# Attention and two feed-forward layers: tables that place each visit in tiles two and three, half-width attention sums, and x's high halves multiplied first

## The chip, the cores and the metric

The kernel runs on one core of one Trainium2 chip. The metric is the device time of one execution in microseconds (us), lower is better. The time before is 940.05 us, the median of 3 runs (938.64 to 941.47).

## The reference, cut to what matters

```python
q_d, k_d, v_d = means of q, k, v over groups of 4 positions       # 144 positions
out_d = softmax(q_d k_d^T / 8) v_d                                # pooled attention
out_local = softmax(q k^T / 8 where |i - j| < 4) v                # banded attention
x = repeat(out_d, 4) + out_local                                  # (4, 8, 576, 64) -> (2304, 512)
h = x @ w1_in;  x = (h * sigmoid(h)) @ w1_out                     # layer 1, 512 -> 2048 -> 512
h = x @ w2_in;  out = (s * relu(h)**2 + b) @ w2_out               # layer 2
```

Batch 4, 8 heads, 576 positions, head width 64, all in fp32.

## The kernel before, in words

**Split products.** Each large product is made of three fp32r matmuls per tile of 128 rows of weights: high half of the weights by high half of the data, high by low, low by high (`PASSES`, line 93). The low half is a subtraction (`split_lo`, line 320, a helper used on DVE and POOL).

**Tiles.** Layer 1 is cut into eight tiles of 288 tokens (half a batch), numbered 0 to 7 in the code (so "tile two" of the title is t = 1). A tile is a list of 32 blocks, `BLOCKS`: up 0, up 1, up 2, down 0, up 3, down 1, ..., up 15, down 13, down 14, down 15. An up block is 12 matmuls of 288 columns into `pH[:, f % 2]` (line 764), a down block 12 matmuls into `pY` (line 769). Four blocks are one **slot**, so that a tile has eight slots of 48 matmuls, and a place in a slot is told by the number `k` of the matmul behind which the small work comes. Layer 2 (line 823 up, line 838 down) has four and a half tiles of 512 tokens, without attention.

**What goes with an up block.** PE finishes up f; ACT takes its tanh (`tanh1`, L909); DVE multiplies (`gate1`, L1195; it signals `g_ready`, for which up f + 2 waits, since it reads pH); ACT rounds the high half (`g_high`, L862); POOL subtracts the low half (`g_low`, L320; it signals `g_split`, for which down f waits).

**Attention beside it.** While tile t is multiplied, the input of tile t + 1 is made. In the start and tile 0, a head has transposes of its probabilities (L621, L625), scores (L599, L602) and sums (`attend`, L645 and L649) on PE; in `small` tile 0 puts the transposes behind matmul 9 of a slot, the scores of the next head behind 15 and the sums behind 38. `attend` multiplies with the pair's two heads at once, so the stationary side has 128 columns, of which 64 are this head's. From tile 1 on only the pooled attention uses PE so. The banded part is done by rows: the scores of a head go to DRAM as bands (`store_band`, `read_band`), and when 8 heads' bands are back, one softmax serves all (`row_shift`, `row_exps`, `row_normalise`); POOL multiplies nine rows of probabilities with v (`weigh`, L1530), DVE sums each (`sum_row`, L1301), PE turns the sums in three groups of three (`turn`, L694), ACT puts a group into x (`place`), DVE adds the pooled part (`x_add`, L1311), ACT rounds the high half (`x_round`) and POOL makes the low half (`x_low`, signals `x1_ready`).

**A visit** is what PE does for one head from tile 1 on (`small_rows`): transposes of the head before, scores of this one, and at each odd head the sums of an earlier pair (`attend_pair`, L663). DVE then takes the maximum (`maxima`), ACT the exponentials and a copy of the scores into the one staging buffer `s_sb` (`exps`), DVE normalises. Tile 1 has 12 visits, tile 2 has 10, tiles 3 to 5 have 8.

**What sets the order.** Every engine runs its own list in order, written out by hand: `UNITS_IN` says which heads a slot of tiles 1 and 2 visits (two per slot in tile 1's first four slots), `TWO_UNITS` at which places (7 and 31), `SOFTMAX_IN` the slot of the row softmax (4 in tile 1), `WEIGH_IN` and `SUM_IN` the slots of the rows, `TURNS_IN` slot and place of the three turns (in tile 1 behind matmuls 36 of slot 6, 2 and 47 of slot 7). In tile 1's last slot (`late`) the steps place, x_add, x_round and x_low stand behind everything else of the tile. Up 0 of a tile waits for `x1_ready` before each chunk of x. The SP queue issues the loads and stores in an order of its own.

## Time and profile before

| what | us |
|---|---|
| median of 3 runs | 940.05 (938.64 to 941.47) |
| the profiled execution's own time | 939.28 |
| its span, first to last instruction | 937.5 |
| its mean granted TensorE clock | 0.998 |
| PE busy | 923.5 (99%) |
| POOL, DVE, ACT busy | 460.6 (49%), 439.5 (47%), 372.8 (40%) |

A busy share counts from an instruction's start to its end; the ends of matmuls are modelled, and consecutive ones overlap. So PE's 99% does not say that PE never waited, and the length of a stage is taken below from starts to starts.

### The profile page before, as it was taken

What the parts mean: (1) busy time and instruction counts of PE and PEld (TensorE: products, weight loads), DVE (VectorE), ACT (ScalarE), POOL (GpSimd) and SP (SyncE); (2) the same over time, 40 slices, a digit from 0 to 9 for tenths busy, and PEclk for the clock granted to TensorE, in tenths of its full rate; (3) what the DMA queues carried; (4) which work ended last, traced back from release to release, by engine and by line L of the source; (5) the groups of instructions that cost most, each with busy time, mean ns of one, the idle gap of its engine ahead of it and who ended that gap; (6) DMA issues with size and microseconds to landing.
All of it is one profiled execution on the core that took longest, in us unless ns stands there. A gap on an engine that the chain in (4) does not pass through costs nothing.

```text
span 937.5 us, 15634 instructions
## 1 busy us (share of the span) xinstructions
PE 923.5 (99%) x5969; PEld 852.0 (91%) x5969; DVE 439.5 (47%) x909; ACT 372.8 (40%) x999; POOL 460.6 (49%) x444
## 2 busy tenths in 40 slices
PE   8999999799999999999999999999999999999998
PEld 8999999799999999999999988888888888888897
DVE  5577436657556566564655642233224222322232
ACT  5666343344534545445345632232224223322332
POOL 7778457859777687685662222213222222222222
PEclk9999999999999999999999999999999999999999
DMA  6756353343442532523006520010002000100000
GB/s 167 196 156 183 76 145 88 84 123 75 96 105 66 136 72 53 143 62 64 22 25 220 162 95 1 1 58 33 0 1 89 0 0 0 67 0 0 35 11 23
DMA packets 87170, 68.75 MB, mean 73 GB/s; under 512 B 38720, under 2 KB 73024, under 8 KB 87104
## 3 DMA queue, kind: packets, MB, share of 16 engines
q1 hardware_dynamic: 86944, 67.71, 27.2%
q8 instruction: 42, 0.69, 0.3%
q14 instruction: 24, 0.20, 0.1%
q10 hardware_dynamic: 160, 0.15, 0.1%
...
## 4 chain that ended last, share of the span: by engine, by line
PE 87%; DVE 5%; ACT 3%; POOL 3%; issue 1%; DMA 1%; ACTq 0%; POOLq 0%; DVEq 0%
PE pH L823 21%; PE pY L838 21%; PE pH L764 17%; PE pY L769 16%; PE pS L599 3%; PE pS L602 2%; PE pO L663 1%; DVE w_in_hl L320 1%; POOL weighted L1530 1%; DMA stage_in<-w_in 1%; PE pO L625 1%; PE pO L649 1%; DVE w_out_hl L320 1%; PE pY L782 1%; POOL g_hl L320 1%
## 5 line engine op out<-in xcount | busy, mean ns | idle before, releaser
L320 POOL TENSOR_TENSOR g_hl<-act,g_hl 128x288 fp32r<-128x288 f32 (+2 forms) x208 | 200.0, 962 | 440.8 <-ACT g_hl L862 440.2
L769 PE MATMUL pY<-g_hl,w_out_hl 128*128 128x288 f32 x1536 | 236.7, 298 | 2.6 <-POOL g_hl L320 2.6
L764 PE MATMUL pH<-x_hl,w_in_hl 128*128 128x288 f32 x1518 | 228.6, 297 | 3.8 <-POOL x_hl L320 3.2
L769 PEld LDWEIGHTS pY<-g_hl,w_out_hl 128*128 128x128 f32 x1536 | 212.0, 188 | 3.5 <-POOL g_hl L320 3.3
L764 PEld LDWEIGHTS pH<-x_hl,w_in_hl 128*128 128x128 f32 x1518 | 209.1, 188 | 4.8 <-issue 3.1
L823 PE MATMUL pH<-x_hl,w_in_hl 128*128 128x512 f32 (+1 forms) x960 | 208.4, 368 | 0.0
L838 PE MATMUL pY<-w_out_hl,g_hl 128*128 128x512 f32 x864 | 207.8, 390 | 0.0
L823 PEld LDWEIGHTS pH<-x_hl,w_in_hl 128*128 128x128 f32 x960 | 169.0, 188 | 31.1
L838 PEld LDWEIGHTS pY<-w_out_hl,g_hl 128*128 128x128 f32 x864 | 161.2, 188 | 33.1 <-POOL g_hl L320 0.3
L1417 DVE TENSOR_TENSOR act<-act 128x512 f32<-128x512 f32 (+1 forms) x80 | 55.5, 694 | 270.6 <-ACT act L1102 270.6
L862 ACT ACTIVATE g_hl<-act 128x288 fp32r<-128x288 f32 (+2 forms) x208 | 104.0, 500 | 191.2 <-DVE act L1419 103.7
L1102 ACT ACTIVATE act<-pH 128x512 f32<-128x512 f32 (+1 forms) x80 | 44.3, 554 | 166.0 <-PE pH L823 165.5
L1530 POOL TENSOR_TENSOR weighted<-p_rows,v_loc 128x896 f32<-128x896 f32 x54 | 91.2, 1692 | 3.2 <-issue 2.1
L909 ACT ACTIVATE act<-pH 128x288 f32<-128x288 f32 x128 | 52.8, 412 | 99.7 <-PE pH L764 99.5
L1195 DVE SCALAR_TENSOR_TENSOR act<-act,pH 128x288 f32<-128x288 f32 x128 | 57.5, 449 | 60.7 <-ACT act L909 59.1
L1301 DVE TENSOR_REDUCE g_gap<-weighted 128x128 f32<-128x896 f32 x36 | 64.3, 1790 | 10.8 <-POOL weighted L1530 10.7
L1484 POOL TENSOR_TENSOR vd_f<-vd_f 72x512 f32<-72x512 f32 x32 | 41.6, 1300 | 6.8 <-DMA vd_f<-vp 6.8
L599 PE MATMUL pS<-qk_f 128*96 128x102 f32 x360 | 43.8, 258 | 0.0
L1419 DVE TENSOR_SCALAR act<-act,sb_col 128x512 f32<-128x512 f32 (+1 forms) x80 | 41.6, 520 | 2.9
L1469 POOL TENSOR_TENSOR pair<-qk_f 128x580 f32<-128x580 f32 x31 | 36.2, 1167 | 5.5 <-DMA qk_f<-qk 3.0
L599 PEld LDWEIGHTS pS<-qk_f 128*96 128x96 f32 x360 | 37.7, 167 | 0.0
L1127 DVE TENSOR_REDUCE pS<-pS 72x1 f32<-72x144 f32 x48 | 14.9, 310 | 44.7 <-PE pS L602 44.7
(141 smaller groups left out, 763.0 us busy)
## 6 DMA issues: line engine op xcount, KB each, us to landing
...
```

What stands on the lines that cost most here:

```text
L320: eng.tensor_tensor(lo, full, hi.bitcast(F32), ALU.subtract).then_inc(signal, 1)
L599: pe.matmul(work(n).s_loc[:, j, :], qk_f[:, buf, q0:q0 + TQ], qk_f[:, buf, c:c + KW], start=not masked_by_pe(n) and j == 0, stop=True, ski ...
L764: last = pe.matmul(pH[:, f % 2, 0:T1], w_in[:, wp, c, f * P:(f + 1) * P], x1[:, par, mp, c, :], start=c + n == 0, stop=c == C - 1 and n == 2)
L769: last = pe.matmul(pY[:, c, 0:T1], w_out[:, wp, f, c * P:(c + 1) * P], g_hl[:, f % RING, mp, 0:T1], start=f + n == 0, stop=f == NF - 1 and ...
L823: last = pe.matmul(pH[:, f % 2, 0:T], w_in[:, wp, c, f * P:(f + 1) * P], x2_hl[:, xp, c, 0:T], start=c + n == 0, stop=c == C - 1 and n == 2)
L838: last = pe.matmul(pY[:, j, :], g_hl[:, f % RING, gp, j * P:(j + 1) * P], w_out[:, wp, f, :], start=f + n == 0, stop=f == NF - 1 and n == 2)
L862: return sc.activation(dst, src, ACT.Copy)
L909: sc.activation(act1[:, f % RING, :], pH[:, f % 2, 0:T1], ACT.Tanh, scale=0.5).then_inc(L[0].t_ready, 1)
L1195: ve.scalar_tensor_tensor(act1[:, f % RING, :], act1[:, f % RING, :], 1.0, pH[:, f % 2, 0:T1], ALU.add, ALU.mult).then_inc(L[0].g_ready, 1)
L1301: ve.tensor_reduce(o_row[i].rearrange("p (h d) -> p h d", h=2), weighted[:, i % 2].rearrange("p (h r d) -> p h d r", h=2, r=NR), AX.X, ALU ...
L1417: ve.tensor_tensor(g, g, g, ALU.mult).then_inc(squared, 1)
L1530: gp.tensor_tensor(weighted[:, i % 2].rearrange("p (h r d) -> p h r d", h=2, r=NR), p_rows[:, i, :].rearrange("p (h r) -> p h r", r=NR).un ...
```

## The change

It does the following; all on the same engines and with the same amount of mathematics.

- Tables (`PLACES_IN`, `QK_PAIRS_IN`, `V_PAIRS_IN`, `SOFTMAX_IN`, `WEIGH_IN`, `SUM_IN`, `TURNS_IN`) give each visit, pair sum, weighed row and turn of tiles 1 and 2 a place. Tile 1's slot 0 visits three heads (behind matmuls 2, 20 and 38), its slot 3 one; the row softmax of tile 1 is at the end of slot 3; turns are groups of 3, 4 and 2 rows in all tiles. One v pair sum passes from tile 1 to tile 2.
- ACT takes the exponentials of a visit before it evacuates a pair.
- `first_up`: up 0 of tiles 1 to 7 multiplies all four high chunks of x with the high weights, then with the low weights, and then the low chunks; `early_ups_end` does the same for the last chunk of tile 0's first two ups, and head 8's sums come right behind it.
- In tile 0 transposes and scores stand together behind matmul 11; `attend` of heads 8 to 15 has only this head's 64 columns on the stationary side and writes partitions 0 to 63. Tanh and gate of ups 0 and 1 are taken together.
- In tile 7, layer 2's up 0 (`up2(0, 0)`) stands ahead of the last down block. ACT waits for `g_split` of all of layer 1 before layer 2's first relu.
- SP issues the v loads behind the band's store instead of ahead of the band's read, and does not ask twice for the same pair.

```diff
-UNITS_IN = {1: [(1, 2), (3, 4), (5, 6), (7, 8), (9,), (10,), (11,), (12,)],
+UNITS_IN = {1: [(1, 2, 3), (4, 5), (6, 7), (8,), (9,), (10,), (11,), (12,)],
...
-SOFTMAX, SOFTMAX_IN = 1, {1: 4, 2: 2}
+SOFTMAX, SOFTMAX_IN = (1, 1), {1: (3, 2), 2: (2, 0)}
...
-GROUP = 3
+GROUPS = ((0, 1, 2), (3, 4, 5, 6), (7, 8))
...
-TURNS_IN = {1: {(6, 36): 0, (7, 2): 1, (7, 47): 2}, 2: {(5, 36): 0, (6, 36): 1, (7, 12): 2}}
+TURNS_IN = {1: {(5, 40): 0, (7, 4): 1, (7, 32): 2}, 2: {(5, 36): 0, (6, 36): 1, (7, 17): 2}}
...
+PLACES_IN = {(1, 0): (2, 20, 38), (1, 1): (9, 34), (1, 2): (8, 31), (1, 3): (17,), (1, 4): (21,),
...
-TRANS_AT, SCORES_AT, ATTEND_AT, LAST_ATTEND_AT, FIRST_ATTEND_AT = 9, 15, 38, 34, 23
+TURN_AT, ATTEND_AT, LAST_ATTEND_AT = 11, 38, 34
...
+HIGH_FIRST = [(0, 0), (1, 0), (0, 1)]
...
+                            if w := unit(h, k + (QK_AHEAD if alone else QK_AHEAD + 1)):
+                                load_qk(w)
                             if w := unit(h, k - 1):
                                 read_band(w)
                             if w := unit(h, k):
                                 store_band(w)
...
+                            if u < H - 1 and (w := unit(h, k + V_AHEAD.get(t, 1))):
+                                load_v(w)
+                        if not alone and len(units(t, u + 1)) == 1:
+                            load_v(unit(h, now[-1] + 1))
...
-                        last = pe.matmul(o.outs[:, HALF:HALF + DQ], vd_s[:, buf, k].rearrange("p h d -> p (h d)"),
-                                         o.pdT[:, k, :], start=k == 0, stop=k == 1, skip_group_check=True)
+                        last = pe.matmul(o.outs[0:D, HALF:HALF + DQ], vd_s[:, buf, k, u % 2], o.pdT[:, k, :],
+                                         start=k == 0, stop=k == 1, skip_group_check=True)
+                    elif not startup(n):
+                        j = k - 2
+                        last = pe.matmul(o.outs[0:D, j * TQ:(j + 1) * TQ], v_f[:, buf, j, u % 2],
+                                         o.pT[:, j * TQ:(j + 1) * TQ], start=False, stop=True, skip_group_check=True)
...
+                def first_up(t, par, h):
+
+                    pe.wait_ge(L[0].g_ready, t * NF + 1)
+                    for n, (wp, mp) in enumerate(HIGH_FIRST):
+                        for c in range(C):
+                            if n == 0 and t == 1:
+                                pe.wait_ge(x_hi, c + 1)
+                            elif n == 0:
+                                pe.wait_ge(x_high, C * (t - 2) + c + 1)
+                            if mp:
+                                pe.wait_ge(x1_ready, C * t + c + 1)
...
+                        if t == N1 - 1 and b == len(BLOCKS) - 1:
+
+                            pe.wait_ge(l.g_ready, s + 2)
+                            up2(0, 0, True, T2)
...
-                    for f in ups[:1]:
+                    together = len(ups) if u == 0 else 1
+                    for f in ups[:together]:
                         tanh1(t, f)
...
+                    if u and any(softmax_in(t, u - 1)[1:]):
                         row_normalise(t, h)
...
+                    if behind:
+                        row_shift(t, h)
```

The same work in the order of the instructions, at three places. The rows give line, operation, output and inputs.

PE in a slot of tile 0 (`pO<-ident` are transposes, `pS` scores, `pO<-pdT` and `pO<-pT` the head's sums), before:

```order
L764 MATMUL pH<-x_hl,w_in_hl 128x288 x10
L621 MATMUL pO<-ident,prob 102x96 x3
L625 MATMUL pO<-ident,prob_d 72x72 x2
L764 MATMUL pH<-x_hl,w_in_hl 128x288 x2
L769 MATMUL pY<-g_hl,w_out_hl 128x288 x4
L599 MATMUL pS<-qk_f 96x102 x3
L602 MATMUL pS<-d_f 72x144
L769 MATMUL pY<-g_hl,w_out_hl 128x288 x8
L764 MATMUL pH<-x_hl,w_in_hl 128x288 x12
L769 MATMUL pY<-g_hl,w_out_hl 128x288 x3
L645 MATMUL pO<-pdT,vd_sum 128x72 x2
L649 MATMUL pO<-pT,v_f 128x96 x3
```

and with the change:

```order
L828 MATMUL pH<-x_hl,w_in_hl 128x288 x12
L666 MATMUL pO<-ident,prob 102x96 x3
L670 MATMUL pO<-ident,prob_d 72x72 x2
L644 MATMUL pS<-qk_f 96x102 x3
L647 MATMUL pS<-d_f 72x144
L833 MATMUL pY<-g_hl,w_out_hl 128x288 x12
L828 MATMUL pH<-x_hl,w_in_hl 128x288 x12
L833 MATMUL pY<-g_hl,w_out_hl 128x288 x3
L690 MATMUL pO<-pdT,vd_sum 64x72 x2
L694 MATMUL pO<-pT,v_f 64x96 x3
```

The scores have joined the transposes, so the large matmuls are broken off twice in a slot and not three times, and the sums write 64 partitions instead of 128.

PE at the seam of tiles 1 and 2 (`pO<-ident,act` is the last turn), with the semaphores that it waits for, before:

```order
L769 MATMUL pY<-g_hl,w_out_hl 128x288 x11
L694 MATMUL pO<-ident,act 128x128 [waits rows_placed,rows_summed,pT_copied,o_copied]
L694 MATMUL pO<-ident,act 128x128
L694 MATMUL pO<-ident,o_last 128x128
L764 MATMUL pH<-x_hl,w_in_hl 128x288 [waits x1_ready,g_ready1]
L764 MATMUL pH<-x_hl,w_in_hl 128x288 x2
L764 MATMUL pH<-x_hl,w_in_hl 128x288 [waits x1_ready]
L764 MATMUL pH<-x_hl,w_in_hl 128x288 x2
L764 MATMUL pH<-x_hl,w_in_hl 128x288 [waits x1_ready]
L764 MATMUL pH<-x_hl,w_in_hl 128x288
L663 MATMUL pO<-pdT,vd_sum 128x144 [waits vd_summed,o_copied,pT_copied,rows_placed]
```

and with the change:

```order
L833 MATMUL pY<-g_hl,w_out_hl 128x288 x11
L795 MATMUL pH<-x_hl,w_in_hl 128x288 [waits x_high,g_ready1]
L795 MATMUL pH<-x_hl,w_in_hl 128x288 [waits x_high] x3
L795 MATMUL pH<-x_hl,w_in_hl 128x288 x4
L714 MATMUL pO<-pdT,vd_sum 128x144 [waits vd_summed,o_copied,pT_copied,rows_placed]
L714 MATMUL pO<-pdT,vd_sum 128x144
L670 MATMUL pO<-ident,prob_d 72x72 [waits pT_copied,probs_ready]
L670 MATMUL pO<-ident,prob_d 72x72
L644 MATMUL pS<-qk_f 96x102 [waits probs_ready,qkd_summed]
L644 MATMUL pS<-qk_f 96x102 x2
L647 MATMUL pS<-d_f 72x144
L795 MATMUL pH<-x_hl,w_in_hl 128x288 [waits x1_ready] x4
```

The last turn is gone from the seam (it stands 15 matmuls earlier), and eight matmuls and a whole visit now come before the first that waits for a low half.

POOL in tile 1 around the first weighed rows (`vd_f`, `vd_sum` a pair sum of v; `pair`, `d_f` one of q and k; `g_hl` is `g_low`), before:

```order
L1484 TENSOR_TENSOR vd_f<-vd_f 72x4x128
L1488 TENSOR_TENSOR vd_sum<-vd_f 72x2x2x64
L320 TENSOR_TENSOR g_hl<-act,g_hl 128x288
L1469 TENSOR_TENSOR pair<-qk_f 128x580
L1473 TENSOR_TENSOR d_f<-pair 128x290
L1530 TENSOR_TENSOR weighted<-p_rows,v_loc 128x896
L320 TENSOR_TENSOR g_hl<-act,g_hl 128x288
L1530 TENSOR_TENSOR weighted<-p_rows,v_loc 128x896 x2
L320 TENSOR_TENSOR g_hl<-act,g_hl 128x288
L1484 TENSOR_TENSOR vd_f<-vd_f 72x4x128
L1488 TENSOR_TENSOR vd_sum<-vd_f 72x2x2x64
L1530 TENSOR_TENSOR weighted<-p_rows,v_loc 128x896
```

and with the change:

```order
L337 TENSOR_TENSOR g_hl<-act,g_hl 128x288
L1576 TENSOR_TENSOR vd_f<-vd_f 72x4x128
L1580 TENSOR_TENSOR vd_sum<-vd_f 72x2x2x64
L1622 TENSOR_TENSOR weighted<-p_rows,v_loc 128x896
L337 TENSOR_TENSOR g_hl<-act,g_hl 128x288
L1622 TENSOR_TENSOR weighted<-p_rows,v_loc 128x896 x2
L337 TENSOR_TENSOR g_hl<-act,g_hl 128x288
L1622 TENSOR_TENSOR weighted<-p_rows,v_loc 128x896
L337 TENSOR_TENSOR g_hl<-act,g_hl 128x288
L1622 TENSOR_TENSOR weighted<-p_rows,v_loc 128x896 x2
L337 TENSOR_TENSOR g_hl<-act,g_hl 128x288
L1622 TENSOR_TENSOR weighted<-p_rows,v_loc 128x896
```

No pair sum stands between the weighed rows any more, and they begin at the start of slot 4 instead of near its end.

## Rows read from the trace of the kernel before

**Rows 1.** Windows of tiles 0 to 3 and 7: span, length, busy by engine, clock, DMA.

```profile
43.70:110.50 66.80, 66.26 (x538) 65.79 (x538) 47.08 (x141) 38.68 (x126) 48.37 (x45) 1.00 0.50 140
...
110.50:182.70 72.20, 66.74 (x535) 65.12 (x534) 42.32 (x97) 29.70 (x99) 49.31 (x49) 1.00 0.48 112
182.70:250.30 67.60, 66.57 (x514) 65.18 (x515) 39.91 (x85) 30.05 (x96) 51.54 (x52) 0.97 0.36 85
250.30:311.50 61.20, 61.20 (x492) 61.10 (x491) 37.43 (x77) 28.15 (x85) 46.48 (x46) 1.00 0.39 92
...
488.00:540.70 52.70, 51.41 (x387) 50.95 (x386) 29.95 (x49) 31.06 (x70) 13.70 (x17) 1.00 0.58 181
```

**Rows 2.** Timeline of PE in tile 1: starts of blocks in slots 4 to 6.

```profile
145.87 1.75 PE L764 MATMUL pH<-x_hl,w_in_hl 128*128 128x288 f32 x12
...
152.05 1.74 PE L769 MATMUL pY<-g_hl,w_out_hl 128*128 128x288 f32 x12
153.63 1.76 PE L764 MATMUL pH<-x_hl,w_in_hl 128*128 128x288 f32 x12
...
160.91 1.76 PE L764 MATMUL pH<-x_hl,w_in_hl 128*128 128x288 f32 x12
```

**Rows 3.** Timeline of PE: three waits, in brackets idle us and releaser.

```profile
49.54 1.59 PE L764 MATMUL pH<-x_hl,w_in_hl 128*128 128x288 f32 x10 [0.51 <-DVE act L1195]
...
182.72 0.64 PE L764 MATMUL pH<-x_hl,w_in_hl 128*128 128x288 f32 x3 [2.91 <-POOL x_hl L320]
...
538.98 1.20 PE L769 MATMUL pY<-g_hl,w_out_hl 128*128 128x288 f32 x7 [1.02 <-POOL g_hl L320]
```

**Rows 4.** Window behind the seam of tiles 1 and 2: granted clock third from the end.

```profile
186.00:188.00 2.00, 2.00 (x13) 2.00 (x12) 0.19 (x1) 0.00 (x0) 0.86 (x2) 0.50 0.00 0
```

**Rows 5.** Timeline of PE in tile 0: a head's sums, a short run, scores.

```profile
90.88 0.56 PE L645 MATMUL pO<-pdT,vd_sum 72*128 72x72 f32 x4
...
91.92 1.43 PE L769 MATMUL pY<-g_hl,w_out_hl 128*128 128x288 f32 x9
...
94.86 0.51 PE L764 MATMUL pH<-x_hl,w_in_hl 128*128 128x288 f32 x2
95.21 0.69 PE L769 MATMUL pY<-g_hl,w_out_hl 128*128 128x288 f32 x4
95.74 0.69 PE L599 MATMUL pS<-qk_f 128*96 128x102 f32 x6
96.26 0.41 PE L602 MATMUL pS<-d_f 128*72 128x144 f32 x2
```

**Rows 6.** Timelines of ACT and DVE at the seam of tiles 1 and 2.

```profile
179.85 0.85 ACT L862 ACTIVATE x_rows<-pO 128x384 f32<-128x384 f32 x1 [3.62 <-PE pO L694]
181.22 1.18 ACT L862 ACTIVATE x_hl<-x_rows 128x288 fp32r<-128x288 f32 x3 [0.52 <-DVE x_rows L1311]
...
180.73 2.16 DVE L1311 TENSOR_TENSOR x_rows<-x_rows,g_gap 128x288 f32<-128x288 f32 x4 [1.44 <-ACT x_rows L862]
```

**Rows 7.** POOL and DVE by form in tile 1: count, busy us, mean ns.

```profile
L1530 POOL TENSOR_TENSOR weighted<-p_rows,v_loc 128x896 f32<-128x896 f32 x9 | 15.1, 1693 | 1.0 <-DVE p_rows L1294 1.0
L320 POOL TENSOR_TENSOR g_hl<-act,g_hl 128x288 fp32r<-128x288 f32 x16 | 12.8, 803 | 16.7 <-ACT g_hl L862 16.6
...
L1301 DVE TENSOR_REDUCE g_gap<-weighted 128x128 f32<-128x896 f32 x6 | 10.5, 1780 | 2.1 <-POOL weighted L1530 2.0
```

**Rows 8.** Timeline of DVE: the row softmax's subtraction in tiles 1 and 3.

```profile
149.93 2.42 DVE L1282 TENSOR_TENSOR e_rows<-e_rows,act 128x126 f32<-128x126 f32 x1
...
263.95 0.40 DVE L1282 TENSOR_TENSOR e_rows<-e_rows,act 128x126 f32<-128x126 f32 x1
```

**Rows 9.** Transfers that touch score_bands in tile 1's first slots.

```profile
DMA to landing us min/median/max: 2.2/3.0/4.2
```

**Rows 10.** Timelines of ACT and POOL: layer 2's first relu and first low half.

```profile
543.61 0.60 ACT L1102 ACTIVATE act<-pH 128x512 f32<-128x512 f32 x1 [2.33 <-PE pH L823]
...
546.33 1.29 POOL L320 TENSOR_TENSOR g_hl<-act,g_hl 128x512 fp32r<-128x512 f32 x1 [7.41 <-ACT g_hl L862]
```

More of the change, by code:

```diff
@@ L962, in slot @@
                         exps(w)
-                    for f in ups[1:]:
+                    for f in ups[together:]:
                         tanh1(t, f)
@@ L1006, in slot_rows @@
                 def slot_rows(t, h, u):
-                    now = units(t, u)
+                    ahead, before, between, after = visits(t, u)
+                    within, at_end, behind = softmax_in(t, u)
                     here = groups(t, u)
-                    two = len(now) == 2
                     finish = u == H - 1 and not late(t, u)
@@ L1017, in slot_rows @@
                         y_out1(t - 1)
+                    for v in ahead:
+                        visit(h, v)
                     f, more = UPS[u][0], UPS[u][1:]
@@ L1021, in slot_rows @@
                         x_round(t, h, 0)
-                    if two:
-                        pooled(h, now[0])
-                        exps(unit(h, now[0]))
+                    for v in before:
+                        visit(h, v)
                     g_high(L[0], t, f, 2, T1)
-                    if u == softmax_in(t) != SOFTMAX:
+                    if within:
                         row_exps(t, h)
@@ L1327, in slot_rows @@
                         x_add(t, h, 0)
-                    if two:
-                        maxima(unit(h, now[0]))
+                    for v in ahead:
+                        maxima(unit(h, v))
+                        normalise(unit(h, v))
+                    for v in before:
+                        maxima(unit(h, v))
                     gate1(t, UPS[u][0])
-                    if u == softmax != SOFTMAX:
+                    for i in sums[1]:
+                        sum_row(t, i)
+                    if within:
                         row_shift(t, h)
```

247 lines of the change are left out of this document (140 added, 107 removed), and 8 rows, old and new, of tables (QK_PAIRS_IN, V_PAIRS_IN).

## The prediction

> **What bounds the kernel now.** The busy times (table above) come first: PE is at work for 99% of the span, no other engine for half of it, so time is only won where PE's own work shrinks or where PE waits. The windows by tile come next [rows 1]. The reader is to see that tile 3 takes 61.2 us and tile 7 52.7, but tile 1 takes 72.2 and tile 2 takes 67.6. To know what they should take, I price a slot from starts [rows 2]. A down block of 12 large matmuls takes 153.63 - 152.05 = 1.58 to 1.59 us, so a slot of four is 6.36. Slot 4, with a visit and a pair's sums, takes 153.63 - 145.87 = 7.76; slot 5, with a visit alone, takes 7.28. So a visit costs 0.92 and a pair's sums 0.48. Tile 1 has 4 visits and one pair more than tile 3: 61.2 + 3.68 + 0.48 = 65.4, and it takes 72.2, so **6.8 us** are lost. Tile 2 has 2 visits and one pair more, 63.5, and takes 67.6: **4.1 us** lost. Tile 7 has 32 blocks only, 50.9, and takes 52.7: **1.8 us**. Tile 0 has one wait of note, 0.51 us [rows 3].
>
> The waits on PE's timeline say where [rows 3]. The largest is 2.91 us at the seam of tiles 1 and 2, for the low half of x, from POOL. Behind it the granted clock falls: a window of 2 us from 186 on has 0.50, the 1.2 GHz level [rows 4]; PE had stood still for 2.91 us before. Over all of tile 2 the clock is 0.97 [rows 1], so 67.6 x 0.03 = 2.0 us of full speed are lost to it, counted within tile 2's 4.1. The rest of tile 1's loss is many small waits and two of 1 us or so in its last slot, where POOL is late. The last large one is 1.02 us before tile 7's last block, for POOL's low half of g [rows 3]. Such a row understates a wait by some 0.15 us, since the end of the matmul before is modelled late.
>
> **The change part by part.**
>
> *Tile 0.* A head's sums take 91.92 - 90.88 = 1.04 us for ten instructions (each fp32 matmul counts twice), 104 ns each, with 72 or 96 columns streamed and 128 columns of weights [rows 5]. The scores stream more, 102 columns, over 96 columns of weights, and take (96.26 - 95.74) / 6 = 87 ns [rows 5]. So the wide weights set the pace, not the stream. With 64 columns of weights the six of 96 streamed columns should take at most 87 ns, and the four of 72 about 87 x 72 / 102 = 61: 0.77 us, 0.27 saved. Bounds: nothing, if something fixed holds it at 104 ns, and 0.5 us, if half the weights meant half the time. I take 0.27, since the scores' row is nearest. Eight heads, all on PE's path: **2.2 us** (0 to 4).
>
> By the Trainium skill (TensorE: Matmul & The Clock Gate, section LDWEIGHTS), a load's time goes with its columns, at 1.2 per ns: 107 ns for 128 and 53 for 64. The 107 agrees with the 104 here; taken alone, the rule would give 0.5 us a head, 4 us in all, and a sum 1.9 us better than mine. I stay with the row, since it counts the stream too.
>
> Breaking off the large matmuls costs something: two of them take 95.21 - 94.86 = 0.35 us where 0.265 is their share [rows 5], so each return costs 0.085. One return fewer in seven slots: **0.6 us**. The scores move 4 matmuls forward and the transposes 2 back; DVE's copy of the transposed probabilities now comes after up f instead of beside it, but the gate behind it is due two blocks later, so that costs nothing. Tanh and gate of ups 0 and 1 are taken together, ahead of head 9's maxima: the 0.51 us (0.66 real) goes. Late next is up 2, with only head 8's shortened sums as cover for tanh and gate of up 0; I leave 0.25 us there. **0.4 us** net. Tile 0: 3.2 us.
>
> *Tile 1.* Nine rows cost POOL 1.69 us each and DVE 1.78, and a `g_low` 0.8 [rows 7]. Before, they shared slots 4 to 7 with three pair sums of 2 us. Now slots 4 and 5 hold seven rows and no pair sum: POOL has 3 x 1.69 + 2 x 0.8 = 6.7 and 4 x 1.69 + 1.6 = 8.4 us for slots of 7.3 to 8.1, and 6.9 in slot 6; `g_low` is due four blocks (6.4 us) after its up, so the excess is hidden. DVE has three sums, 5.3 us, in each of slots 5 and 6, and beside them at most 2.7 us: tile 3's 37.4 busy us less nine sums, over eight slots [rows 1, 7]. That is 8.0 for slots of 7.6 and 7.8, but the gates are due two blocks (3.2 us) later. What is late next: the q and k sum of head 12, last in slot 6 on POOL, about 0.3 us; and slot 0, where three visits stand 18 matmuls apart, 2.4 + 0.9 = 3.3 us. Each visit must copy its scores into the one staging buffer after the store of the last has landed, median 3.0, up to 4.2 us [rows 9]. I leave 0.6 us there. Some 0.2 more for other small waits: 1.1 us.
>
> *The seam of tiles 1 and 2.* Before, from the last turn ACT's place took 0.85 us from 179.85, then x_add, x_round and x_low held PE to 182.72 [rows 3, 6]. The last turn has moved from behind matmul 47 to behind 32, 15 matmuls or 2.0 us earlier, and places two rows, not three. From the turn, place (an estimate of 0.65 for two rows), x_add (2.16 / 4 = 0.54) and x_round (0.45) [rows 6] with signals bring the first high chunk after 2.1 us: PE comes then. The four high chunks follow each other at 0.5 us, PE needs 0.13 each: about 1.1 us of waiting in small pieces. Then come four matmuls without a wait and a visit with a pair's sums, 1.9 us, under which POOL makes the low halves. I take **1.3 us** for the seam, (0.5 to 3), and no fall of the clock, because no single stop is near 2.9 us; tile 7, with its stop of 1.02, has a clock of 1.00 [rows 1].
>
> *Tile 2.* The visits are spread (7, 31, then 9, 40), and the last turn stands at 17 instead of 12; 0.4 us of small waits stay. So of 6.8 + 4.1 = 10.9 us of loss, 1.1 + 1.3 + 0.4 = 2.8 remain: **8.1 us** saved.
>
> *Tile 7.* Up 0 of layer 2 takes 2.7 us and covers the last `g_low`: **1.1 us**. The last down block now ends later against layer 2's first relu, but the relu still has two up blocks (5.4 us) before down 0 needs it; the chain from relu to the end of `g_low` takes 546.33 + 1.29 - 543.61 = 4.0 us [rows 10]. Covered, with the relu waiting for ACT's four copies of y first.
>
> *Tiles 3 to 6.* `first_up` changes nothing where x is ready. Group two now turns four rows, so place is about 0.3 us longer, hidden by the 15 matmuls (2 us) before the next turn. The v loads stand behind the band's store, some 4 us later in a slot, and are read in the next one. The SP queue's other waits stay. Cost nothing; if these covers failed, a few tenths per tile.
>
> The sum: 3.2 + 8.1 + 1.1 = **12.4 us**. The profiled execution took 939.28 us (span 937.5), so the changed one should take 926.9; the median of the runs shown is 0.8 above it, so 940.05 - 12.4 = **927.7 us**.
>
> **The rivals.**
>
> *POOL blocks the row softmax and the weighed rows slide.* The same subtraction took 0.40 us in tile 3 and 2.42 in tile 1, where POOL ran without a pause [rows 8]. The change puts it at the end of slot 3, where a v pair sum follows `g_low` on POOL. SP also issues the read of band 7 only behind a v load that waits for POOL's pair sum in slot 3. If both add up to 4 us, rows and turns slide by as much and the seam opens again: about 4 us of the 8.1 are lost, **931.7 us**. Against: `g_low`'s slack takes up the first 2 us, which I counted. The Trainium skill (SBUF — State Buffer, Who interferes with whom) says that a DVE instruction with two SBUF inputs and a POOL one that reads SBUF exclude each other for a whole instruction, which is what these rows look like and speaks against placing it there.
>
> *The clock falls at the seam again*, because four short stops act as a long one: 2.0 us stay, **929.7**.
>
> *The narrow weights bring nothing*: a fixed cost per fp32 pass, 2.2 us stay, **929.9**.
>
> *Slower.* The row softmax stands in DVE's list ahead of slot 4's gates. If band 7 lands late, everything on DVE waits, and with it PE's ups, one for one. Expected is landing before slot 4 begins; slack is about 4 us. To end 2.8 us above the time before it would have to cost 15 us, landing 19 us late. That decides it, and with landings of 2.2 to 4.2 us [rows 9] it would need a queue of four or five of them in series on SP. Then **943 us** or more.
>
> **How the numbers follow.** Forecast 0.63, POOL 0.13, clock 0.11, weights 0.07, slower 0.03, and 0.03 for a change whose tables mostly fail, with only tile 0 and tile 7 kept and new waits, near the old time. A measurement can tell 0.3%, 2.8 us, from no change: faster is under 937.2. So faster 0.94, same 0.03, slower 0.03. The range: the best end takes a seam of 0.5 and 1 us more from the weights and small waits, 924.7; the upper one holds POOL's case with 2 us of tile 0 lost too, 933.7.
>
> **What would show it.** Right: tile 0 at 63.6 us with a head's sums near 0.77; tile 1 near 66.5, tile 2 near 65; no wait of PE over 1 us at the seam, clock 1.00 in it; tile 3 still 61.2; no wait before tile 7's last down. Wrong: waits for `prob_d` in slot 0, a subtraction of over 2 us that moves the first weighed row behind 5 us of slot 4, or a seam of over 2 us.

## The result, and the profile after

The changed kernel takes 933.05 us (median of 4 runs, 932.34 to 933.89). The kernel before took 940.76 us in the 4 runs made beside it (938.64 to 941.55). The ratio is 0.9932, with a 95% interval of 0.9917 to 0.9947. So it is faster: the medians differ by 7.7 us, and the interval of the ratio stands for 5.0 to 7.8 us, where 12.4 were forecast. The profiled execution took 932.44 us with a span of 930.6, 6.9 us less than the span of before.

Where did the rest of the 12.4 us go? The starts of PE's first matmul of each tile answer it. Tile 0 counts from its first matmul behind the start-up (43.70 us before, 43.57 after); tile 7 ends where layer 2's first down block starts.

| stretch, us | before | after | difference | forecast |
|---|---|---|---|---|
| tile 0 | 66.81 | 68.09 | +1.28 | -3.2 |
| tiles 1 and 2 | 72.21 + 67.57 | 66.75 + 64.91 | -8.12 | -8.1 |
| tiles 3 to 5 | 61.20, 61.22, 61.22 | 61.86, 61.86, 61.84 | +1.92 | 0 |
| tile 6 | 54.05 | 54.05 | 0 | 0 |
| tile 7 | 60.87 | 59.10 | -1.77 | -1.1 |
| start-up, and layer 2 from its first down block | 432.4 | 432.1 | -0.2 | 0 |

The same windows as in [rows 1], of the changed kernel (columns as there: span, then busy of PE, PEld, DVE, ACT and POOL, clock, DMA share, GB/s):

```profile
43.57:111.66 68.09, 65.73 (x541) 63.03 (x539) 51.75 (x142) 37.57 (x126) 47.93 (x46) 1.00 0.51 143
111.66:178.41 66.75, 66.34 (x536) 65.23 (x534) 39.15 (x96) 30.30 (x98) 46.53 (x46) 1.00 0.41 102
178.41:243.32 64.91, 64.59 (x513) 63.61 (x514) 39.99 (x86) 30.90 (x98) 52.55 (x53) 1.00 0.42 104
243.32:305.18 61.86, 61.45 (x492) 61.11 (x490) 37.73 (x79) 28.66 (x87) 48.71 (x49) 1.00 0.37 91
```

Tile 2's clock is back at 1.00 (0.97 before). DVE is busy 51.75 us in tile 0, 4.7 more than before, with one instruction more: its instructions got longer. The timeline of PE shows the waits that are left (in brackets idle us and releaser):

```profile
68.63 0.43 PE L666 MATMUL pO<-ident,prob 96*102 96x96 f32 x3 [0.93 <-DVE x_f L1263]
87.43 0.43 PE L666 MATMUL pO<-ident,prob 96*102 96x96 f32 x3 [1.42 <-DVE x_f L1263]
178.41 1.94 PE L795 MATMUL pH<-x_hl,w_in_hl 128*128 128x288 f32 x8 [0.20 <-ACT x_hl L938]
303.49 1.85 PE L833 MATMUL pY<-g_hl,w_out_hl 128*128 128x288 f32 x12 [0.41 <-POOL g_hl L337]
```

The 2.91 us at the seam [rows 3] are 0.20 now, and the 1.02 us before tile 7's last block are gone. New are two waits in tile 0 (2.35 us together, about 0.15 more for each in fact, as in the prediction) and one of 0.32 to 0.41 before the last down block of tiles 2 to 5. Follow the 1.42 back: the transposes wait for DVE's `x_f`, and DVE is late from here on:

```profile
75.21 0.45 DVE L1263 TENSOR_TENSOR x_f<-pO,o_down 64x288 f32<-64x288 f32 x1 [0.62 <-ACT o_down L938]
75.70 3.42 DVE L1269 CAST x_hl<-x_f 128x288 fp32r<-128x288 f32 x1
79.15 0.86 DVE L337 TENSOR_TENSOR x_hl<-x_f,x_hl 128x288 fp32r<-128x288 f32 x1
```

The same cast takes 0.31 to 0.73 us at its three other places. POOL's timeline over the same stretch has no pause between its first four instructions, and one of 0.07 us (78.95 to 79.02) ahead of the fifth:

```profile
74.54 1.29 POOL L337 TENSOR_TENSOR w_out_hl<-stage_out,w_out_hl 128x512 fp32r<-128x512 f32 x1
75.79 0.80 POOL L337 TENSOR_TENSOR g_hl<-act,g_hl 128x288 fp32r<-128x288 f32 x1
76.56 1.28 POOL L337 TENSOR_TENSOR w_out_hl<-stage_out,w_out_hl 128x512 fp32r<-128x512 f32 x1
77.80 1.15 POOL L1561 TENSOR_TENSOR pair<-qk_f 128x580 f32<-128x580 f32 x1
79.02 0.67 POOL L1565 TENSOR_TENSOR d_f<-pair 128x290 f32<-128x290 f32 x1
```

The cast ended at 79.12, just behind that pause. Before, POOL had a gap of 0.26 us at 75.3 there and one of 0.62 behind its `g_low`, and the cast took 0.31.

The sums of a head, on PE and on its weight loads (PEld), beside [rows 5]:

```profile
54.68 0.56 PE L833 MATMUL pY<-g_hl,w_out_hl 128*128 128x288 f32 x3
55.16 0.47 PE L690 MATMUL pO<-pdT,vd_sum 72*64 72x72 f32 x4
55.47 0.66 PE L694 MATMUL pO<-pT,v_f 102*64 102x96 f32 x6
56.06 1.46 PE L833 MATMUL pY<-g_hl,w_out_hl 128*128 128x288 f32 x9
```

```profile
55.16 0.32 PEld L690 LDWEIGHTS pO<-pdT,vd_sum 72*64 72x64 f32 x4 [0.17 <-issue]
58.81 0.34 PEld L666 LDWEIGHTS pO<-ident,prob 96*102 96x102 f32 x3
```

From 55.16 to 56.06 the ten instructions take 0.90 us, not 0.77. The three large matmuls ahead take 0.48, not the 0.39 of the kernel before: the first load of 64 columns comes only when its matmul is due, with 0.17 us in which PEld does nothing. The second group of narrow loads, at 55.41, is ahead of its matmul (55.47) again. The load of the 102-column transposes, at 58.81, comes 0.13 us ahead of its matmul at 58.94.

### The profile page after: what moved, and what is told of

It reads as the page before. It is cut to its first block, busy times and chain, and to the rows that moved or that the text cites. A ratio compares the mean times of both kernels' runs of the same rounds, so it can differ in the third digit from the quotient of the medians.

```text
span 930.6 us, 15634 instructions
## 1 busy us (share of the span) xinstructions
PE 920.2 (99%) x5969; PEld 847.5 (91%) x5969; DVE 440.2 (47%) x909; ACT 372.9 (40%) x999; POOL 460.1 (49%) x444
## 4 chain that ended last, share of the span: by engine, by line
PE 85%; POOL 5%; DVE 3%; issue 2%; ACT 2%; DMA 1%; SPq 1%; ACTq 0%; POOLq 0%; DVEq 0%
PE pH L897 21%; PE pY L912 21%; PE pY L833 16%; PE pH L828 16%; PE pS L644 3%; POOL weighted L1622 2%; POOL g_hl L337 1%; PE pS L647 1%; PE pH L795 1%; PE pO L714 1%; POOL vd_f L1576 1%; PE pY L856 1%; PE pO L670 1%; POOL vd_sum L1580 1%; DVE act L1276 0%
## 5 line engine op out<-in xcount | busy, mean ns | idle before, releaser
L828 PE MATMUL pH<-x_hl,w_in_hl 128*128 128x288 f32 x1428 | 212.2, 296 | 0.0
L897 PEld LDWEIGHTS pH<-x_hl,w_in_hl 128*128 128x128 f32 x960 | 169.0, 188 | 30.9
L828 PEld LDWEIGHTS pH<-x_hl,w_in_hl 128*128 128x128 f32 x1428 | 196.1, 188 | 0.2 <-DVE act L1276 0.2
L946 ACT ACTIVATE pS<-pS,stats 72x144 f32<-72x144 f32 x60 | 20.7, 345 | 43.0 <-DVE stats L1211 32.5
```

What stands on the lines that cost most here:

```text
L828: last = pe.matmul(pH[:, f % 2, 0:T1], w_in[:, wp, c, f * P:(f + 1) * P], x1[:, par, mp, c, :], start=c + n == 0, stop=c == C - 1 and n == 2)
L897: last = pe.matmul(pH[:, f % 2, 0:T], w_in[:, wp, c, f * P:(f + 1) * P], x2_hl[:, xp, c, 0:T], start=c + n == 0, stop=c == C - 1 and n == 2)
```

## The experiments

Lengths of tile 0 are counted in this section from the start of up 2, the one mark that is the same in all kernels; by it the kernel before has 64.89 us and the change 66.18. The table has the profiled executions (us); "net" is tile 0 less its listed waits, each counted 0.15 us longer than its row says. For the kernel before, with its one wait of 0.51, the net is 64.23. e7, e8 and e9 also have e3's edit, and e12 is e9 with one more.

| kernel | tile 0 | net | tiles 1 + 2 | tile 3 | tile 7 | time, median |
|---|---|---|---|---|---|---|
| the change | 66.18 | 63.53 | 131.66 | 61.86 | 59.10 | 933.05 |
| e1, groups of 3, 3, 3 | 65.96 | 63.54 | 132.90 | 61.18 | 60.04 | 932.99 |
| e2, wide weights | 64.90 | 64.26 | 132.25 | 61.84 | 60.17 | 932.87, one run |
| e3, ACT casts | 63.48 | 63.48 | 132.39 | 61.86 | 60.06 | 931.68 |
| e4, split | 66.02 | 63.89 | 131.93 | 61.84 | 61.26 | 934.77, one run |
| e5, halves mixed | 65.02 | 63.52 | 136.07 | 61.86 | 61.20 | 937.17, one run |
| e6, mask first | 65.71 | 63.55 | 131.84 | 61.87 | 60.97 | 933.12, one run |
| e7, 72 columns | 61.88 | 61.39 | 131.60 | 61.87 | 59.11 | 929.73, one run |
| e8, cast and groups | 63.49 | 63.49 | 131.77 | 61.22 | 59.10 | 928.39 |
| e9, e8 and 72 columns | 61.90 | 61.39 | 131.67 | 61.18 | 60.80 | 926.00 |
| e10, reduction | 64.99 | 63.51 | 131.70 | 61.85 | 60.03 | 932.30, one run |
| e11, last turn later | 64.93 | 63.53 | 133.46 | 61.86 | 60.22 | 934.07, one run |
| e12, x later | 61.86 | 61.36 | 131.98 | 61.18 | 60.56 | 928.40 |

**e1: groups of three rows again.**

```diff
-GROUPS = ((0, 1, 2), (3, 4, 5, 6), (7, 8))
+GROUPS = ((0, 1, 2), (3, 4, 5), (6, 7, 8))
```

> The changed kernel with turns of 3, 3 and 3 rows again; all else stays. Theory: the group of four rows makes ACT's place 1.18 us long instead of 0.9, so that tanh, g_high and g_low of up 14 start about 0.4 us later, POOL gives the last low half 0.66 us later, and PE waits 0.41 us (0.56 real) before the last down block. Then tiles 3 to 5 (61.86 us each) go back to 61.2, the wait before their last down block is gone, tile 2 gains 0.5 too, the seam of tiles 1 and 2 loses up to 0.3 since the last group has three rows again: 2.2 us less in all, with a ratio to the kernel before near 0.991. Rival, the v loads that stand behind the band's store are the cause: tiles 3 to 5 stay at 61.8 and the time stays within 0.3 us.

Tiles 3 to 5 took 61.18, 61.23 and 61.22: the theory for them holds, and the v loads are cleared. The chain shows in both timelines. The copy of the four rows pushes tanh of up 14 to 296.73, 53.41 us into tile 3, where e1 has it at 52.99, and the last low half ends 0.67 us later in the tile (60.11 us into it, against 59.44). The rows are place and that low half, of the change and then of e1:

```profile
295.78 1.18 ACT L938 ACTIVATE x_rows<-pO 128x512 f32<-128x512 f32 x1 [1.46 <-PE pO L744]
302.43 1.00 POOL L337 TENSOR_TENSOR g_hl<-act,g_hl 128x288 fp32r<-128x288 f32 x1
```

```profile
296.79 0.91 ACT L938 ACTIVATE x_rows<-pO 128x384 f32<-128x384 f32 x1 [1.35 <-PE pO L744]
302.89 1.02 POOL L337 TENSOR_TENSOR g_hl<-act,g_hl 128x288 fp32r<-128x288 f32 x1
```

But the whole kernel gained nothing (932.99): with three rows in the last turn the seam waits 0.23 + 0.57 us, and tile 2's last down block 0.55, so tiles 1 and 2 took 1.2 us more, not 0.2 less as I had summed; tile 7 took 0.9 more, for a reason of its own (below). The two groupings suit different tiles.

**e2: wide weights again.**

```diff
-    o.outs[0:D, j * TQ:(j + 1) * TQ], v_f[:, buf, j, u % 2], ...
+    o.outs[:, j * TQ:(j + 1) * TQ], v_f[:, buf, j].rearrange("p h d -> p (h d)"), ...
```

(the same for `vd_s`, and ACT and DVE read the head's own rows)

> The changed kernel with the sums of heads 8 to 15 over 128 columns of weights again. Theory: the narrow weights bring 0.90 instead of 1.04 us a head, but the first narrow load stands 0.17 us idle behind the 128-column ones and the three matmuls ahead of it take 0.48 instead of 0.39, so 0.06 us a head and 0.4 to 0.5 us in eight heads: tile 0 gets 0.4 to 0.5 us longer (68.5), a slot without waits 8.65 instead of 8.59. Rival, the forecast's own price, whose gain only hides behind late DVE work in tile 0: 0.27 us a head, a slot without waits 8.86, tile 0 near 70.2.

A slot without waits takes 8.65 us (53.21 to 61.86), against 8.59 of the change (53.10 to 61.69): beside the merged transposes and scores, the narrow weights bring 0.06 us a head, not 0.27.

```profile
53.21 1.75 PE L828 MATMUL pH<-x_hl,w_in_hl 128*128 128x288 f32 x12
61.86 1.75 PE L828 MATMUL pH<-x_hl,w_in_hl 128*128 128x288 f32 x12
```

Net, tile 0 is 0.7 us longer, of which 0.5 are waits that no row lists: two of its slots take 8.97 and 8.84 us. Yet tile 0 as a whole is 1.3 us *shorter* than the change's, since it met 0.49 us of waits instead of 2.35. My expectation of +0.4 was wrong in sign: the waits decide, not PE's work.

**e3: ACT rounds the high half in tile 0.**

```diff
-                        ve.tensor_copy(x1[:, par, 0, c, :], x_f[:]).then_inc(x_hi, 1)
+                        sc.wait_ge(x_summed, n + 1)
+                        copy(x1[:, par, 0, u // 2, :], x_f[:]).then_inc(x_hi, 1)
```

> The changed kernel; in tile 0 ACT rounds the high half of x (x_f to x1) instead of DVE, and DVE makes the low half a few instructions later. Theory: the wait of 1.42 us before the transposes at 87.43 us comes from the one rounding on DVE that took 3.42 us at 75.70, beside POOL instructions without a gap, where others took 0.31 to 0.73; on ACT it takes 0.45, DVE is never 2.8 us late, the wait of 1.42 goes and tile 0 takes 66.5 us (1.6 less); the wait of 0.93 at 68.63 stays, because that one comes from a subtraction for w_in of 1.64 us. Rival: the slot is too full for DVE in any case, with the edge mask's memsets (1.1 us) in it: the wait stays over 1 us and tile 0 at 68.1.

Tile 0 fell from 66.18 to 63.48, with no wait left, not even the 0.93. That is 2.7 us where 1.6 were expected. The kernel took 931.68 us (928.81 to 933.26), ratio to before 0.9905 (0.9870 to 0.9940). That is 1.4 us under the change's median, with ranges that overlap; in its profile tile 7 and tiles 1 and 2 took 1.7 us more than in the change's.

**e4: transposes and scores apart.**

```diff
-                    if k == TURN_AT and u:
+                    if k == 9 and u:
                         trans_unit(unit(h, u))
+                    if k == 15 and u:
                         score_unit(unit(h, u + 1))
```

> The changed kernel with the transposes of tile 0 behind matmul 9 and the scores behind 15 again. Theory: the merge brings 1.18 - 1.07 - 0.09 = 0.03 us a slot and 0.2 us in seven, but it also moves DVE's copy of the probabilities behind up f. So split, a slot without waits takes 8.62 and tile 0 changes by -0.5 to +0.3 us, because waits may move. Rival, the forecast's price: 0.085 a slot, tile 0 0.6 us longer.

A slot takes 8.65 (53.34 to 61.99), and tile 0 net 0.36 us more: beside narrow weights the merge is worth 0.06 a slot and 0.4 in all, between theory and rival. The rows are those of e4, then of the kernel before:

```profile
53.34 1.75 PE L829 MATMUL pH<-x_hl,w_in_hl 128*128 128x288 f32 x12
61.99 1.75 PE L829 MATMUL pH<-x_hl,w_in_hl 128*128 128x288 f32 x12
```

```profile
88.90 1.75 PE L764 MATMUL pH<-x_hl,w_in_hl 128*128 128x288 f32 x12
97.56 1.75 PE L764 MATMUL pH<-x_hl,w_in_hl 128*128 128x288 f32 x12
```

So e2 and e4 must not be added up. The kernel before, which has neither the narrow weights nor the merge, takes 8.66 a slot. Either of the two alone (e2 and e4) leaves 8.65, and both together 8.59: 0.07 us a slot in all, 0.5 in tile 0.

**e5: halves mixed again in up 0.**

```diff
-                            first_up(t, par, h)
+                            first_up_mixed(t, par, h)
```

(`first_up_mixed` waits per chunk for `x1_ready` and then does the three `PASSES`)

> The changed kernel with up 0 of tiles 1 to 7 in the old order (high, low, high by low, chunk by chunk, each chunk waiting for its low half). Theory: POOL gives the four low halves of tile 2 from 178.34 us on at 0.87 us each, so PE starts at 179.2 and each chunk waits; the visit behind matmul 7 fills one gap. Up 0 with its visit ends at 182.9 instead of 182.0: 0.9 us longer in tile 2 with waits of 0.4 to 0.9 us for POOL's x_hl, nothing in the others (x is ready there), and no fall of the clock. Rival, the order is what closed the seam (2.91 us before): over 2 us longer and the clock at 0.50 behind it.

The theory fell, the rival holds. PE stood still for 1.50 us:

```profile
177.88 2.28 PE L808 MATMUL pH<-x_hl,w_in_hl 128*128 128x288 f32 x8 [1.50 <-POOL x_hl L337]
```

After it the granted clock was at 0.50 for 6 us. Windows of PE behind the seam (clock third from the end):

```profile
178.00:180.00 2.00, 1.86 (x9) 1.40 (x10) 0.00 (x0) 0.76 (x3) 2.00 (x4) 0.80 0.83 241
180.00:182.00 2.00, 2.00 (x12) 1.94 (x12) 0.00 (x0) 0.00 (x0) 1.80 (x3) 0.50 0.94 201
182.00:184.00 2.00, 2.00 (x11) 2.00 (x10) 0.47 (x2) 0.10 (x1) 0.00 (x0) 0.50 0.24 69
184.00:186.00 2.00, 2.00 (x10) 2.00 (x9) 1.14 (x4) 1.93 (x8) 0.00 (x0) 0.50 0.55 129
```

Tiles 1 and 2 took 136.07 instead of 131.66: 4.4 us, of which 1.3 lie before tile 2's first matmul (the stop) and 3.1 behind it (six microseconds at half the clock). High halves first is more than half of what the two tiles gained. This rests on one profile of e5; its one time, 937.17, is 4.1 us above the change's median. It also shows that tile 0, whose code is untouched here, takes 65.02 where the change's profile has 66.18: the cast at this place took 0.83 us, and the listed waits are 1.15 us shorter.

**e6: the edge mask ahead of the start-up's sums.**

```diff
                 for u in range(H):
                     slot(h, u, 0, True)
-                    if u == H // 2:
-                        set_edges()
...
+                set_edges()
                 first_sums()
```

> The changed kernel with the edge mask's memsets at the start of DVE's list, where DVE is idle for 2.2 us, instead of in tile 0's slot 4. Theory: DVE is 2.8 us late there from one rounding of 3.42 us, and the memsets (85.72 to 86.84 us) come on top, so the wait of 1.42 before the transposes at 87.43 shrinks by 1.1 to about 0.3, if that rounding takes as long again; tile 0 near 67.0. Since e2 and e4 show that the waits of tile 0 change with small shifts, the longest rounding may also take another time; then the row of that rounding tells. Rival, the memsets cost nothing because ACT's copy of the pooled part is what x_f waits for: wait stays 1.4.

The long cast came again (3.40 us at 74.84), so the case is the right one. The wait before the transposes fell from 1.42 to 0.91, not to 0.3. DVE stood ready 1.1 us sooner, but now waited 0.62 us for ACT's `o_down`. Half of the theory, half of the rival.

**e7: 72 columns of weights instead of 64.**

```diff
-    v_f[:, buf, j, u % 2]
+    v_f[:, buf, j].rearrange("p h d -> p (h d)")[:, 0:72]
```

(the same for `vd_s`)

> The kernel of e3 (ACT rounds in tile 0) with 72 columns of weights instead of 64 in the sums of heads 8 to 15; the odd heads take the even head's values, so their sums are not the reference's. Theory: what costs 0.17 us of idle weight load is the step from weights of over 64 columns to 64 columns and back (transposes with 102 and 72 columns are loaded ahead without a gap), so with 72 the first load comes ahead, the three matmuls before take 0.39 again, and the ten instructions take 0.8 to 0.85 us: a slot without waits takes 8.4 instead of 8.59, tile 0 gets 1.4 us shorter (62.1 where e3 has 63.5 by the same marks). Rival, any narrowing has that gap, because the load waits for its data or for the group before: a slot takes 8.59 to 8.65 and tile 0 stays.

The theory holds: the gap is gone, and the gain is above what was expected. PE and PEld in a slot of tile 0:

```profile
56.29 0.55 PE L833 MATMUL pY<-g_hl,w_out_hl 128*128 128x288 f32 x3
56.68 0.42 PE L690 MATMUL pO<-pdT,vd_sum 72*72 72x72 f32 x4
56.94 0.66 PE L694 MATMUL pO<-pT,v_f 102*72 102x96 f32 x6
57.38 1.44 PE L833 MATMUL pY<-g_hl,w_out_hl 128*128 128x288 f32 x9
```

```profile
56.55 0.40 PEld L690 LDWEIGHTS pO<-pdT,vd_sum 72*72 72x72 f32 x4
```

The three matmuls ahead take 0.39, the load comes 0.13 us ahead of its matmul, and the ten instructions take 0.70 us: 1.04 wide, 0.90 with 64 columns, 0.70 with 72. A slot takes 8.30. Eight columns *more* save 0.29 us a slot, 0.35 against wide.

**e8: e3 and groups by tile.**

```diff
+                    group = (GROUPS_EARLY if t in (1, 2) else GROUPS)[g]   # 3, 4, 2 or 3, 3, 3 rows
```

> The kernel of e3 (ACT rounds in tile 0), with turns of 3, 3 and 3 rows in tiles 3 to 5 and of 3, 4 and 2 in tiles 1 and 2. Theory: the terms add, since they lie in different tiles: tile 0 as in e3 (2.7 us shorter than the change), tiles 3 to 5 61.2 instead of 61.86 (1.9 in all), tiles 1 and 2 as in the change within 0.6, tile 7 at 60.0 as in e1 to e3. So 4.6 us off the change's own 933.05, less up to 1 in tile 7: 928.5 to 929.5, ratio to the kernel before 0.988. Rival, tiles 3 to 5 pay elsewhere what they gain: 930.5 or more.

Both terms add: 63.49 and 61.22, and 928.39 us (927.63 to 929.65), ratio 0.9888 (0.9869 to 0.9907).

**e9: e8 with 72 columns for the right head.**

```diff
-        v_f = sb("v_f", [KW, 2, NJ, 2, D], F32, early)
+        v_wide = sb("v_f", [KW, 2, NJ * 2 * D + 8], F32, early)
...
+                        at = (2 * j + u % 2) * D
+                        last = pe.matmul(o.outs[0:72, j * TQ:(j + 1) * TQ], v_wide[:, buf, at:at + 72],
```

> The kernel of e8 with 72 columns of weights in the sums of heads 8 to 15, now with the right head: the buffers of v and of its sums get 8 columns more at their end, so that a slice of 72 columns can start at either head; the 8 rows too many are never read. To make room, the rows of the softmax take the place of a filler, and their first load waits for the low half of x in tile 0. Theory: as in e7, a slot of tile 0 without waits takes 8.30 instead of 8.59, 0.29 us in each of eight slots: 2.3 us off tile 0 of e8, so 926.1 us where e8 had 928.39, ratio to the kernel before 0.986. Rival: with less of PE's time to cover them, DVE and POOL come late in tile 0 again (e7 had one wait of 0.34) and half of it is lost: 927.3.

926.00 us (925.57 to 927.81), ratio 0.9851 (0.9835 to 0.9868), as expected: 13.8 us under the kernel before beside it, 1.8 times the gain of the change. It is the best version here.

**e10: the rounding as a reduction.**

```diff
-                        ve.tensor_copy(x1[:, par, 0, c, :], x_f[:]).then_inc(x_hi, 1)
+                        ve.tensor_reduce(x1[:, par, 0, c, :], x_f[:].unsqueeze(2), AX.X, ALU.max).then_inc(x_hi, 1)
```

> The changed kernel; the rounding of x_f stays on DVE at its place, but as a reduction over an axis of one element instead of a cast. Theory: the cast took 3.4 us in three executions, where POOL's instructions followed each other without a gap, and 0.3 to 0.8 elsewhere, since as a cast it needs what POOL holds; a reduction takes 0.4 to 0.5 us in all four places whatever POOL does, the wait of 1.42 before the transposes is under 0.3, and tile 0 takes 64.6 to 64.9 us by the marks by which the change has 66.18. Rival, any DVE instruction that reads and writes SBUF there waits for POOL: one of the four takes over 1 us.

The most instructive miss. DVE and POOL at the critical place:

```profile
74.94 0.45 DVE L1269 TENSOR_REDUCE x_hl<-x_f 128x288 fp32r<-128x288 f32 x1
75.43 3.02 DVE L337 TENSOR_TENSOR x_hl<-x_f,x_hl 128x288 fp32r<-128x288 f32 x1
78.37 1.16 DVE L337 TENSOR_TENSOR w_in_hl<-stage_in,w_in_hl 128x512 fp32r<-128x512 f32 x1
```

```profile
74.96 0.82 POOL L337 TENSOR_TENSOR g_hl<-act,g_hl 128x288 fp32r<-128x288 f32 x1
75.73 1.29 POOL L337 TENSOR_TENSOR w_out_hl<-stage_out,w_out_hl 128x512 fp32r<-128x512 f32 x1
76.97 1.16 POOL L1561 TENSOR_TENSOR pair<-qk_f 128x580 f32<-128x580 f32 x1
78.21 0.77 POOL L1565 TENSOR_TENSOR d_f<-pair 128x290 f32<-128x290 f32 x1
```

The reduction took 0.45 us at all four places, whatever POOL did. But the subtraction behind it, with two inputs in SBUF, then stood 3.02 us, and PE waited 1.33 us all the same. (The first wait, 0.93 us in the change, was gone.) The subtraction ended at 78.45, not at the end of POOL's row (78.98) but, like the cast of the change, behind a pause of 0.08 us ahead of POOL's last instruction. So a cast and a subtraction are both shut out; the wait is a matter of which DVE instruction meets a row of POOL instructions without a gap. Such a row does not always hold DVE up to its end: in e5 POOL's rows show no pause either behind the `g_low` at this place, and the cast got in there after 0.83 us, with POOL's next instruction 1.35 us long instead of 1.28. What decides between the two stays open. In e3 it was luck in part: there POOL left 0.05 us between two instructions, the subtraction for w_in got in and took 1.06 us, the next one 1.53, and POOL waited instead (1.64 us for an instruction of 1.29).

**e11: tile 1's last turn twelve matmuls later.**

```diff
-TURNS_IN = {1: {(5, 40): 0, (7, 4): 1, (7, 32): 2}, ...
+TURNS_IN = {1: {(5, 40): 0, (7, 4): 1, (7, 44): 2}, ...
```

> The changed kernel with tile 1's last turn behind matmul 44 of its last slot instead of 32. Theory: twelve matmuls later are 1.59 us, all of which PE then waits at the seam: a stop of 1.7 to 1.8 us instead of 0.2, and, since e5 with a stop of 1.50 had the clock at 0.50 from 180 to 186 us, the clock falls here too: tile 2 gets 2 to 3 us longer on top, 3.6 to 4.6 in both tiles. Rival, e5's fall came from PE working with short stops in the four chunks after the long one, which high halves first don't have: 1.6 us in both tiles and a clock of 1.00.

The rival holds, nearly. The stop was 1.38 us with another of 0.57 behind three matmuls, tiles 1 and 2 took 133.46 (+1.8), and the clock stayed at 1.00:

```profile
178.00:180.00 2.00, 1.16 (x4) 0.67 (x5) 1.36 (x3) 1.47 (x5) 1.80 (x3) 1.00 0.82 225
180.00:182.00 2.00, 2.00 (x20) 1.99 (x20) 0.00 (x0) 1.04 (x4) 2.00 (x4) 1.00 0.99 210
```

The turn's place is worth about 0.15 us a matmul. A stop of 1.38 us left the clock alone, one of 1.50 did not; whether the length alone or what stood around it decides stays open.

**e12: layer 2's input loaded later.**

```diff
                 for f in range(WSLOTS):
                     load_in(1, f)
-                load_x2(0, 2)
...
+                    if f == 4:
+                        load_x2(0, 2)
```

> The kernel of e9 with the first load of layer 2's input (x_f<-x_scratch, 1 MB, 9.3 us to landing) issued after the weights of four ups of layer 2 instead of after two. Theory: the same code of tile 7 took 59.1 to 61.3 us in the profiles so far, and it goes with how long ACT waited for the third piece of layer 2's weights, whose transfer shares the queue's time with that load: waits of 1.3 to 1.6 us go with 59.1, of 2.9 to 3.2 with 60.0 to 60.2, of 3.8 to 4.4 with 60.8 to 61.3. With the large load later, the wait is under 1.5 us and tile 7 takes 58.6 to 59.1 us: 924.5 us where e9 had 926.0, and a spread of runs under 1.5 us; ratio to the kernel before 0.984. Rival: the wait moves to another piece or x2's high half comes late in the middle of the tile, and tile 7 stays at 60 us or more.

A miss: 928.40 us (924.87 to 929.16), tile 7 at 60.56. The wait moved, to `stage_out` pieces (2.09 and 1.76 us on ACT), and the spread grew. What the profiles do show is that the length of tile 7 goes with ACT's wait for a weight piece that has yet to land; the shortest and the longest of e1 to e11 are those of e8 and e4:

```profile
487.80 0.63 ACT L939 ACTIVATE w_in_hl<-stage_in 128x512 fp32r<-128x512 f32 x1 [1.29 <-DMA stage_in<-w_in]
```

```profile
495.46 0.63 ACT L939 ACTIVATE w_in_hl<-stage_in 128x512 fp32r<-128x512 f32 x1 [4.36 <-DMA stage_in<-w_in]
```

With 1.29 tile 7 takes 59.10, with 4.36 61.26, and PE then waits 1.27 us for a gate. In this way single profiles of the same code differ by 2 us. That the wait is the cause is argued from this agreement in the twelve profiles of the change and e1 to e11, not shown: the one run made to shorten it moved it instead.

## Why the prediction was right for tiles 1 and 2 and wrong for the rest

The forecast was 927.7 us and the time is 933.05. What failed is the terms of tile 0 (two mis-sized, one left out) and the cover named for tiles 3 to 5. That 933.05 lies within the stated range is luck: its upper end, 933.7, was made of 4 us for POOL's case, which did not come, and of 2 us lost in tile 0. The lower end was also added up wrongly (927.7 less 0.8 for the seam and less 1 is 925.9, not 924.7), and the rule for weight loads, taken alone, makes 4 - 2.2 = 1.8 us, not 1.9.

**Tiles 1 and 2 (8.1 forecast, 8.12 measured): right in mechanism, with luck in the digits.** Tile 1 was forecast near 66.5 and took 66.75, tile 2 near 65 and took 64.91. POOL's row of weighed rows kept pace, tile 1's slot 0 waits 0.20 us for one `prob_d`, and the row softmax cost nothing: its subtraction took 0.66 us in tile 1, and 2.40 in tile 2 as before, with no wait of PE behind it. The seam was forecast at 1.3 us of waiting in small pieces and shows 0.20: PE's 15 matmuls behind the last turn cover nearly all of place, x_add and x_round, and the roundings of ACT then come 0.4 us apart. What I missed at the seam is how near it stood to the clock's fall: e5 prices high halves first at 4.4 us, of which I had given it none by itself. Since the seam came 1.1 us better than summed, other small losses came as much worse, and most of them are in no row: the listed waits of the two tiles are 0.20, 0.20 and 0.32 us where 2.8 remain. The other 3.7 of the 8.12 us, the tables' part, were not taken apart by a run.

**Tile 0 (3.2 forecast, 1.3 us longer instead): wrong, in three terms.** Net of the waits on both sides tile 0 gained 0.7 us by the mark of up 2 (64.23 to 63.53).

- *"With 64 columns of weights the six ... should take at most 87 ns"*: mis-sized. 2.2 us were forecast; 0.5 came beside the merge (e2), and 0.1 without it (e4 against the kernel before). The row of the scores was nearest in columns streamed, but has 96 columns of weights; a price taken from it holds for e7 with 72 columns (0.35 a head, better than my 0.27), not for 64. With 64 the first load isn't made ahead. The Trainium skill (TensorE: Matmul & The Clock Gate, section Part 3: Packing small matmuls — row/col tiling) says that PE pulls a weight load ahead of matmuls under way when it goes to rows that don't conflict or to the background buffer. The trace agrees for 72, 96, 102 and 128 columns, whose loads start up to 0.13 us ahead of their matmuls. It does not for the first load of 64 columns behind those of 128, which starts with its matmul at 55.16.
- *"each return costs 0.085. One return fewer in seven slots: 0.6 us"*: mis-sized as well: 0.4 came beside the narrow weights (e4), 0.1 without them (e2 against the kernel before). Neither brings much without the other, and of the 2.8 us of both steps 0.5 came, 0.07 us a slot. Why they come only together stays open.
- *"Late next is up 2 ... I leave 0.25 us there"*: the sum had no term for DVE in tile 0. DVE's casts and subtractions meet POOL's in every slot, and I priced them as if they had fixed lengths. New waits of 2.65 us (1.4 to 2.65 in the six profiles with this tile's work unchanged but for the edits of e6 and e10) came from there; with the cast on ACT (e3, e8) there was none. I had the rule in hand, at the row softmax [rows 8], and applied it only to tile 1. The Trainium skill (SBUF — State Buffer, Who interferes with whom) names `cast` with the instructions that can take the pair of ports shared with GpSimd, and says that a reduction never contends on trn2. The traces agree: 3.42 us for the cast in the change, 0.45 for the reduction in e10. They also agree with its sentence on two SBUF inputs (3.02 us for the subtraction in e10). But the prediction took from it a lock for a whole instruction, and these stalls reached over three and four instructions of POOL.

The terms close: of 3.2 forecast, take 2.3 off for the two steps, add 0.25 that up 2 did not need, add 0.2 for a wait of the kernel before that no PE row lists (its third slot takes 8.88 us, not 8.66), and take off 2.65. That gives 1.3 us longer, as measured. The PEld row of the kernel before at that wait:

```profile
68.48 0.26 PEld L621 LDWEIGHTS pO<-ident,prob 96*102 96x102 f32 x3 [0.24 <-issue]
```

**Tiles 3 to 5 (0 forecast, 1.9 us longer): wrong.** The step said "place is about 0.3 us longer, hidden by the 15 matmuls (2 us) before the next turn". The price was right, 1.18 against 0.91 us, but the cover named was the wrong one. What stands behind place on ACT is tanh and `g_high` of up 14, and behind those POOL's v sums, `x_low` and the last `g_low`, which had ended just in time. Each engine's next instruction has to be followed, not only the one that reads the result. The "few tenths per tile" of the failed cover was 0.66, three times.

**Tile 7 (1.1 forecast, 1.77 in the profile):** the early up 0 removes the last wait as said. The 0.7 us beyond are chance: the other profiles of the same code have 59.1 to 61.3, and before had 60.87 with its 1.02 us wait.

**Rivals.** POOL blocking the row softmax and a falling clock at the seam did not come, nor did the late band. "The narrow weights bring nothing" came nearly true in its price (0.1 to 0.5 of 2.2 us), but not by its mechanism: a fixed cost would have held 72 columns too, and these brought 0.35 a head (e7). The two losses in tile 0 and in tiles 3 to 5 no rival held. They are the same fault: I looked for the loss in tile 1, where the change was large, and not where it was small.
